# Expert rows turned by VectorE instead of TensorE, loaded in blocks; the expert tables moved into the branch

## The reference, cut to what matters

```python
x = attn_out.transpose(0, 2, 1, 3).reshape(3072, 512)
logits = x @ w_gate                    # 8 experts
expert_idx = np.argmax(logits, axis=1)
for e in range(8):
    mask = expert_idx == e
    h = np.maximum(x[mask] @ w1[e], 0.0)      # 512 -> 1024
    out[mask] = gate_w[mask, None] * (h @ w2[e])   # 1024 -> 512
h = out @ w_in                         # 512 -> 2048
g = (a0 + a1 h + a2 h^2 + a3 h^3) / (1 + |b0| |h| + |b1| h^2 + 1e-6)
y = g @ w_out                          # 2048 -> 512
```

## Time and profile before

| what | value |
|---|---|
| median of three runs | 1128.35 us |
| the profiled execution's own time | 1129.99 us |
| its span, first to last instruction | 1128.4 us |
| TensorE busy | 1095.0 us (97%) |
| VectorE busy | 896.5 us (79%) |
| ScalarE busy | 594.8 us (53%) |
| GpSimd busy | 259.7 us (23%) |
| mean granted TensorE clock | 0.995 of full speed |

### The profile page before, as it was taken

One profiled execution on the slowest core, in us unless ns is written; L12 is line 12 of the kernel. 1 busy time (PEld: TensorE's weight loads), 2 busy tenths in 40 slices (PEclk: granted clock), 3 DMA queues, 4 the chain that ended last, 5 costly groups with the idle time before them and its releaser, 6 DMA issues.

```text
span 1128.4 us, 19524 instructions
## 1 busy us (share of the span) xinstructions
PE 1095.0 (97%) x6023; PEld 890.5 (79%) x6024; DVE 896.5 (79%) x1810; ACT 594.8 (53%) x1063; POOL 259.7 (23%) x191
## 2 busy tenths in 40 slices
PE   6999999989999999999999999999999999999997
PEld 4677777678888888888887888888888888888885
DVE  5688788658878787878769987986986986996975
ACT  5788888422322222232338656655665655655663
POOL 1112111255646656563500001001001001000101
PEclk9999999899999999999999999999999999999999
DMA  8998861287757877975721010010002001000000
GB/s 196 310 240 215 225 169 59 71 280 262 269 193 274 278 249 240 305 233 201 258 94 49 1 39 38 1 38 37 0 0 76 0 0 64 12 0 10 28 1 38
DMA packets 142363, 142.54 MB, mean 126 GB/s; under 512 B 104672, under 2 KB 104672, under 8 KB 141280
## 3 DMA queue, kind: packets, MB, share of 16 engines
q0 software_dynamic: 27584, 92.48, 23.5%
q1 hardware_dynamic: 114720, 49.31, 16.3%
HBM read 118.70 MB, written 23.32 MB: 126 GB/s over the span
## 4 chain that ended last, share of the span: by engine, by line
PE 84%; DVE 8%; SPq 3%; DMA 2%; issue 2%; ACT 1%; POOL 0%; POOLq 0%; ACTq 0%; DVEq 0%
PE bank L1122 23%; PE bank L1124 23%; PE bank L1123 23%; PE bank L969 4%; PE bank L945 3%; PE bank L932 3%; DMA qraw<-in_q_dram 2%; PE bank L910 1%; PE bank L1117 1%; PE bank L985 1%; DVE poly L1726 1%; DVE poly L1724 1%; PE bank L1192 1%; DVE poly L1739 1%; SPq L316 1%
## 5 line engine op out<-in xcount | busy, mean ns | idle before, releaser
L1612 DVE STREAM_TRANSPOSE bank<-hbuf 32x256 f32<-32x256 f32 x464 | 211.6, 456 | 61.9 <-ACT hbuf L745 55.5
L469 POOL TENSOR_TENSOR w_lo<-stage,w_hi 128x2048 fp32r<-128x2048 f32 x32 | 147.6, 4614 | 64.9 <-DMA w_hi<-in_moe_w_dram 32.1
L1122 PE MATMUL bank<-w_hi,gh 128*128 128x512 f32 x384 | 150.5, 392 | 0.3 <-DVE gl L1748 0.3
L1122 PE MATMUL bank<-x2Th,w_hi 128*128 128x512 f32 x384 | 149.5, 389 | 0.5 <-DVE poly L1726 0.5
L1124 PE MATMUL bank<-w_hi,gl 128*128 128x512 f32 x384 | 149.5, 389 | 0.0
L1123 PE MATMUL bank<-w_lo,gh 128*128 128x512 f32 x384 | 149.4, 389 | 0.0
L1124 PE MATMUL bank<-x2Th,w_lo 128*128 128x512 f32 x384 | 149.4, 389 | 0.0
L1123 PE MATMUL bank<-x2Tl,w_hi 128*128 128x512 f32 x384 | 149.4, 389 | 0.0
L604 POOL DMA_INDIRECT out_dram<-stage,ids x24 | 29.6, 1235 | 510.1 <-ACT stage L854 494.3
L1122 PE MATMUL bank<-w_hi,xTh 128*128 (+1 forms) x248 | 96.7, 390 | 2.2 <-DVE xTl L1600 1.5
L756 ACT ACTIVATE ybuf<-bank 128x512 f32<-128x512 f32 x31 | 18.5, 598 | 149.8 <-PE bank L1124 141.8
(11 more groups left out here) (220 smaller groups left out, 2222.6 us busy)
## 6 DMA issues: line engine op xcount, KB each, us to landing
w_hi<-in_moe_w_dram POOLq DMA_DIRECT2D x32, 1024.0 KB, 7.8
stage<-in_moe_w_dram POOLq DMA_DIRECT2D x32, 1024.0 KB, 7.8
xg<-routed_x SPq DMA_DIRECT2D x31, 256.0 KB, 5.1
routed_y<-ybuf SPq DMA_DIRECT2D x31, 256.0 KB, 2.8
x<-routed_y SPq DMA_DIRECT2D x6, 1056.0 KB, 5.2
kraw<-in_k_dram SPq DMA_DIRECT2D x24, 256.0 KB, 5.1
qraw<-in_q_dram SPq DMA_DIRECT2D x24, 256.0 KB, 4.1
vraw<-in_v_dram SPq DMA_DIRECT2D x24, 256.0 KB, 4.1
```

Source lines behind the costliest of these rows:

```text
L469: pool.tensor_tensor(w_lo[:, at:at + CH], stage[:, c % 2, :], w_hi[:, at:at + CH].bitcast(F32), ALU.subtract).then_inc(chunk_ready, 1)
L1122: pe.matmul(dst, lhs_hi, rhs_hi, start=first, stop=False)
L1612: ins = dve.transpose(HB_ps[k][r * QD:(r + 1) * QD, :, q % 2 * QD:(q % 2 + 1) * QD], rows)
```

## The change

1. TensorE no longer turns x. VectorE does it with one `transpose` over 128x512, which turns each block of 32x32 within its 32 partitions. For this to be the whole turn, the loads place the blocks: each tile is loaded by four DMAs (`load_rows`), one for each group of 32 partitions, with four pieces of 128 columns per partition, and the columns of a row in `xs` stand in another order. `turn_x` writes them in that order (`quarters`), and the reciprocals of the sums are laid out to match it (`rcp` with 16 entries a tile, a `den` for the sums).
2. The turn of x of tile t+1 stands first in VectorE's `dve_tile(t)`. Tile 1 has places of its own (`XS_ps`, `xSh`, `xSl`).
3. The expert tables are a function, called at the end of each branch, and hold the turns of x0 and x1 and both low parts of x behind `tab_ready`. TensorE waits for `tab_ready` ahead of the up products of tile 0, and makes half of the up products of tile 1 before it turns h0. TensorE's loop has one tile per round, VectorE's two.
4. GpSimd waits for 64 instead of 16 at `xg_in[0]`.

```diff
+            def load_rows(r, row):
+                for a in range(4):
+                    sp.dma_start(xg[a * QD:(a + 1) * QD, r, :].rearrange("n (b c) -> n b c", b=4),
+                                 xs[ds(row, P), a * P:(a + 1) * P].rearrange("(b n) c -> n b c", b=4)).then_inc(xg_in[r], 16)
+
             def load_x(t, r, first=False):
...
-                sp.dma_start(xg[:, r, :], xs[ds(row, P), 0:DM]).then_inc(xg_in[r], 16)
+                load_rows(r, row)
...
-            moe_x(0)
-            moe_h(0); moe_x(1); end_ht(0, hTh)
+            moe_x(0); moe_x(1, XS_ps, xSh)
+            moe_h(0); end_ht(0, hTh)
...
+            def quarters(row, j):
+
+                return row.rearrange("p (a j n) -> p a j n", a=4, j=KB)[:, :, j, :]
...
-                    mm = pe.transpose(dst[:, j * P:(j + 1) * P], oT[:, i % 2, j, :], ident[:, :])
+                    mm = pe.transpose(quarters(dst[:, :], j), oT[:, i % 2, j, :], ident[:, :])
...
-            def moe_turn_x(r, n):
-
-                pe.wait_ge(xg_in[r], 16 * n)
-                for j in range(KB):
-                    mm = pe.transpose(X_ps[:, j * P:(j + 1) * P], xg[:, r, j * P:(j + 1) * P], ident[:, :])
-                mm.then_inc(xg_ps, 1)
...
-            def pe_tile(t, r, n):
+            def pe_tile(t):
...
-                moe_turn_x(r, n)
                 moe_down(t - 1, off_down, e_down)
                 moe_up(t + 1, off_up, e)
...
-            moe_turn_x(0, 1)
-            moe_up(0, 0, 0)
             pe.wait_ge(tab_ready, 1)
             off, e = weights_at(1), expert_of(1)
-            moe_turn_x(1, 1)
+            moe_up(0, 0, 0)
+            moe_up(1, off, e, xSh, xSl, (0,))
             turn_end_h(0)
-            moe_up(1, off, e)
-            pe_tile(1, 0, 2)
-            with pe.Fori(0, (MT - 3) // 2) as tp:
-                for r in range(2):
-                    pe_tile(2 * tp + r + 2, (r + 1) % 2, tp + r + 2)
+            moe_up(1, off, e, xSh, xSl, (1,))
+            pe_tile(1)
+            with pe.Fori(2, MT - 1) as t:
+                pe_tile(t)
...
-                dve.tensor_tensor(xt[:, i % QT, 0:DM].rearrange("p (h d) -> p h d", h=H),
-                                  src[:, :].rearrange("p (h d) -> p h d", h=H),
-                                  rcp[:, i % 2, 1, :].rearrange("p (h o) -> p h o", o=1).broadcast_to([P, H, D]),
+                dve.tensor_tensor(xt[:, i % QT, 0:DM].rearrange("p (s n) -> p s n", n=QD),
+                                  src[:, :].rearrange("p (s n) -> p s n", n=QD),
+                                  rcp[:, i % 2, :, :, :].rearrange("p u v (j o) -> p (u v j) o", o=1).broadcast_to([P, 16, QD]),
...
+            def turn_rows(t, r, n, dst=X_ps):
+
+                dve.wait_ge(xg_in[r], 64 * n)
+                if dst is X_ps and not (isinstance(t, int) and t == 0):
+                    dve.wait_ge(xg_lo, t)
+                dve.transpose(dst[:, :].rearrange("p (j b n) -> p j b n", j=KB, b=4),
+                              xg[:, r, :].rearrange("p (b j n) -> p j b n", j=KB, b=4)).then_inc(xg_ps, 1)
+
+            def expert_tables():
...
+                dve.tensor_copy(end_i[:, :, :], edge[:, 2:4, :]).then_inc(tab_ready, 1)
+                turn_rows(0, 0, 1); turn_rows(1, 1, 1, XS_ps)
+                moe_x(0); moe_x(1, XS_ps, xSh, xSl)
...
             with dve.If(banded(dve) > 0):
                 dve_steps()
+                expert_tables()
...
-            def dve_tile(t):
-                turn_h(t, 0); moe_x(t + 1); turn_h(t, 1); moe_ht(t)
-
-            moe_x(1); end_ht(0, hTh, hTl)
-            with dve.Fori(1, MT - 2) as t:
-                dve_tile(t)
+            def dve_tile(t, r, n):
+                turn_rows(t + 1, r, n); turn_h(t, 0); moe_x(t + 1); turn_h(t, 1); moe_ht(t)
+
+            end_ht(0, hTh, hTl)
+            with dve.Fori(0, (MT - 3) // 2) as tp:
+                for r in range(2):
+                    dve_tile(2 * tp + r + 1, r, tp + 2)
+            turn_rows(MT - 1, 0, MT // 2 + 1)
```

More of the change, by code:

```diff
@@ L139, in build_program @@
         sums = over("sums", [P, 2, H])
-        rcp = over("rcp", [P, 2, 2, H])
+        den = over("den", [P, 2, H])
+        rcp = over("rcp", [P, 2, 2, 2, KB])
         zeros = over("zeros", [P, RW])
@@ L163, in build_program @@
         early = free[1]
+        x2_at = free[1]
         x2 = over("x2", [P, G, RW])
+        xSh, x2_at = place("xSh", [P, KB, P], F32R, x2_at)
+        xSl, _ = place("xSl", [P, KB, P], F32R, x2_at)
         x2Th = over("x2Th", [P, KB, G * P], F32R)
@@ L194, in build_program @@
         HT_ps = bank[2:4]
+        XS_ps = bank[6]
         HB_ps = [bank[2 + k].rearrange("p (j n) -> p j n", j=FB) for k in range(2)]
@@ L675, in evac_logits, with head_cols @@
                 act.activation(lgT[:, :], X_ps[:, 0:P], ACT.Copy).then_inc(lt_sb, 1)
+            def head_cols(row, h):
+                return row.rearrange("p (u v j n) -> p u v j n", u=2, v=2, j=KB)[:, h % 2, :, h // 2, :]
             def normalise_last():
@@ L1124, in three, with moe_up @@
                 return pe.matmul(dst, lhs_lo, rhs_hi, start=False, stop=last)
-            def moe_up(t, off, e):
+            def moe_up(t, off, e, hi=xTh, lo=xTl, halves=(0, 1)):
                 pe.wait_ge(chunk_ready, e * 4 + 2)
                 pe.wait_ge(xg_lo, t + 1)
-                for n in range(2):
+                for n in halves:
                     if not isinstance(t, int) or t > 0:
@@ L1135, in moe_up @@
                         at = off + j * F + n * 512
-                        mm = three(H_ps[n][:, :], xTh[:, j, :], xTl[:, j, :], w_hi[:, ds(at, 512)], w_lo[:, ds(at, 512)],
+                        mm = three(H_ps[n][:, :], hi[:, j, :], lo[:, j, :], w_hi[:, ds(at, 512)], w_lo[:, ds(at, 512)],
                                    j == 0, j == KB - 1)
@@ L1563, in _ @@
                     low_part(n // 4, n % 4)
-            done[0] = 0
-            tl = lambda ins: link(ins, tab_step)
-            dve.wait_ge(count_ps, 1)
-            tl(dve.tensor_copy(expert_rows[:, :], X_ps[:, 0:E]))
-            per_tile = lambda x: x.rearrange("p (s o) -> p s o", o=1).broadcast_to([P, MT, E])
-            per_expert = lambda x: x.rearrange("p (o e) -> p o e", o=1).broadcast_to([P, MT, E])
-            tl(dve.tensor_tensor(more, expert_rows[:, :].rearrange("p (e o) -> p e o", o=1).broadcast_to([P, E, NT]),
-                                 steps[:, :].rearrange("p (o j) -> p o j", o=1).broadcast_to([P, E, NT]), ALU.is_gt))
@@ L1590, in _ @@
-            for k in range(2):
-                tl(dve.tensor_tensor(prod[:, k, :, :], past, per_expert(wide[:, 0, k, :]), ALU.mult))
-            tl(dve.tensor_reduce(ttab[:, 0:2, :], prod[:, 0:2, :, :], AX.X, ALU.add))
-            tl(dve.tensor_tensor(ttab[:, 0, :], ttab[:, 0, :], row_no[:, :], ALU.add))
-            tl(dve.scalar_tensor_tensor(out=ttab[:, 2, :], in0=ttab[:, 1, :], scalar=last_at[:, 0:1], in1=ttab[:, 0, :],
-                                        op0=ALU.add, op1=ALU.min))
```

100 lines of the change are left out of this document (57 added, 43 removed).

## The result

The changed kernel takes 1132.76 us (median of 17 runs, 1130.96 to 1136.04) where the kernel before takes 1129.2 us (17 runs on the same chip, 1126.42 to 1131.19). The ratio is 1.0035, 95% interval 1.0027 to 1.0042: slower by a third of a per cent. The prediction was 1119.2 us, faster by 0.8%. It is wrong, in size and in sign. The profiled execution took 1132.76 us, its span is 1130.8 us.

The account below looks back on a forecast made before the run. The prediction took TensorE, with no gap to fill, to bound the expert stage. Loop -13.0 us and start-up +3.8 us summed to -9.2 us, from a median of 1128.35 to 1119.2 us, range 1113.5 to 1125.5.

Parts of the forecast that it names:

- What bounds the kernel: Expert stage: TensorE is busy 342.5 of 343.0 us; time saved there counts only while no other engine ends later.
- The loop, TensorE: Expert loop: x's transposes leave TensorE, 27 at 0.48 us, -13.0 us; bounds -13.5 and -9.5.
- The loop, VectorE: Expert loop: one added 0.73 us transpose per tile fits VectorE's wait for relu, 10.37 of 10.87 us; costs nothing.
- the estimate of 1.24 us: VectorE's transpose of x: four times the skill's 311 ns per 128x128 bf16, which would leave VectorE no slack.
- The loads: Loop: four DMAs of 512 B pieces per x tile instead of one; x is read two periods later; costs nothing.
- Attention stage: Before the expert stage: another column order and 16 reciprocals for 8, at most 24 x 0.01 us on VectorE; nothing.
- The start-up: Routing to first down product: earlier tables, but x1's landing and half clock delay TensorE; +3.8 us, bounds -1.5 to +9.
- The end: Stage's end: removing the last transpose (x30) buys nothing, as TensorE already waits 0.43 us there for VectorE; 0 us.
- A: Start-up rival: the clock stays up or x1 comes early; -12 us, 1116 us; chance 0.17.
- B: Loop rival: VectorE sets the pace, by a 1.2 to 1.6 us transpose or thin 0.4 us slack; about 1124; chance 0.14.
- C: Start-up rival: VectorE's 4.25 us gap before the tables stays; total -4.5 us, 1124 us; chance 0.09.
- D: Loop rival: VectorE's transpose runs its four quadrants in turn, 3.74 us; +60 us, 1188 us; chance 0.07.

Follow-up runs that it names:

- e6: Changed kernel with TensorE's four value reads split around the down products and only 8 of 128 columns per block of x's low part computed in the loop; ratio 0.9931.
- e8: Changed kernel with split reads, x0's low part before x1's turn, weights behind x1, x's low part earlier among h's transposes, 20 fillers for 8; 1110.89 us, ratio 0.9865.
- e1: Changed kernel with the two values that only the up products need read behind the down products; ratio 0.9991 to the kernel before.
- e7: Changed kernel with one more, unused value read per tile on TensorE's sequencer, ahead of the down products; 1141.65 us, ratio 1.0129 to the kernel before.
- e12: Kernel before the change with one more, unused value read per tile on TensorE's sequencer, ahead of the transposes; 1137.18 us, ratio 1.0068.
- e10: Kernel before the change with TensorE's four value reads split over the two borders of a tile; ratio 0.9995.
- e2: Changed kernel with only 8 of 128 columns per block of x's low part computed in the loop, the rest left out; ratio 0.9984 to the kernel before.
- e11: Changed kernel with 56 instead of 8 filler products on TensorE in the last group, behind the branch; ratio 1.0033 to the kernel before.
- e5: The changed kernel itself, unaltered, run again on another call's chip; 1131.10 us, ratio 1.0043 to the kernel before.
- e3: Changed kernel in which VectorE, at the start of the expert stage, makes x0's low part before it turns x1; ratio 0.9991 to the kernel before.
- e9: Kernel before the change with only the expert tables, coef and x0's low part moved inside the branch, x still turned by TensorE; ratio 1.0018.
- e4: Changed kernel in which GpSimd starts the second expert's weight loads only when x1 has landed too; ratio 1.0007 to the kernel before.

## Why the prediction was wrong

*What bounds the kernel: right as far as it went.* TensorE had no gap to fill. But "only while no other engine ends later" was weighed with engines alone. The holder that turned up is a sequencer, whose work no busy share counts.

*The loop, TensorE: the step that failed.* "The transposes go", priced at 0.48 us each with 27 of them, -13.0 us, and at least -9.5. The transposes are worth 0.50 us a tile (e6, e8), so the price was right; the step from "they go" to "the period falls by their price" failed. 3.8 us came of 13.0. The sequencer's branch and four reads hold the down products (S: e1 gives back 0.17 us a tile; e7 and e12, against e10), and x's low part holds the up products (e2 gives back 0.12); both mended together give 0.38. The prediction asked what covers the work that is added, and never what the removed work had been covering. It also put at nothing, without a word, that TensorE's loop now branches in every tile instead of every second one, 0.4 us of the sequencer each time.

The Trainium skill ("Advanced Engine Details and Errata", Sequencer and Instruction Queues, Control Flow Timing) gives some 108 ns for a compare-and-branch; this trace has 213 ns. The Trainium skill ("DMA: Bandwidth & Descriptors", Latency and other measured facts) gives a floor of about 600 ns for a `tensor_load`; the trace has 0.30 us for the load, and about 0.7 us from one read to the next with the register operations around it. The measured numbers decide. Four reads by that figure would be an estimate of 2.4 us; by the trace, about 3. Either number, beside the 3.7 us which the trace of before shows between a branch and the last up product (341.6 to 345.24), would have been a reason to ask.

*The loop, VectorE: right, but for one operand.* 0.73 us predicted and measured, and the estimate of 1.24 us beside it was not borne out; the transpose stands in the wait for the relu, of which 0.7 to 1.0 us are left. The 0.4 us before the down products were more than enough (1.0 us in the tile shown). Only the up products' low part was not on the list.

*The loads: right in the loop.* No tile waits for an x there. *Attention stage: right*, nothing to see beyond its spread.

*The start-up: the steps right, one size off.* (Its sum is +3.6, not +3.8: 243.8 + 2.7 - 242.86. That changes nothing below.) Tables at once, row_i 5.5 us behind them (215.20 to 220.57 + 0.18), both low parts behind x1, the clock at its lower level, and 2.8 us lost by it (2.7 predicted; e11, though e5 lost 1.9). Missed: x1's landing. "I take 2.7 to 3" was 6.12 us. SP issued x1 8.6 to 10.5 us behind the last routing step (223.92 and 225.81, less 215.29), for 8.6 to 10.3 predicted. The weights were put at 10.2 us behind it and came at 9.6 (224.91 - 215.29), while x1 was still being issued, so the two collided as they do in the kernel before: the earlier trace rows showed 6.82 us for it, and I argued myself away from that row with a lead of a few tenths. x1's turn came 16.7 us after the last routing step (231.96 - 215.29) for 13.0 predicted, 3.7 us that cover the miss of 3.4 (+7.2 for +3.8).

*The end: 0.8 us where I had 0,* by the low part of the last x.

*The rivals.* A (clock up): no, 0.50. B (VectorE the pace): no; the loop's gain came a little below its lower end (-3.8 for -5 to -10), but neither of its two mechanisms is there: the transpose takes 0.73 us, and the low part of h is ready a microsecond early. VectorE did hold products, the up products, by the low part of x, which B doesn't name; that it was near in number is luck. C (the gap stays): no. D (3.74 us for the transpose): no. The result is slower than before, which I gave 0.08, and the mechanism that took the gain was in none of the rivals. Had x1 landed as predicted, the change would have been about even (+2.4 - 3.4 + 1.9 = +0.9 us in the profiled executions), not -9.2. Had the loop come as predicted and x1 late, it would still have been some 6 us faster (-9.2 + 3.4). So the error in the loop took the gain, and the one in the start-up made a loss of it.

## What to carry to other kernels

Before an operation is taken out of a saturated engine's stream, list what its duration may cover: the sequencer's branches, value reads and waits at that point, and every operand due right behind it; a profile without gaps says nothing of how near they are. Where two of them are near, neither mend alone shows its worth, so try them together. Put value reads behind the products that don't need them, and start bulk transfers behind the last small one that a critical step waits for.

## What the runs showed of the hardware

- One value read on TensorE's sequencer is a load of 0.30 us (least 0.296, most 1.1 over the loop), register operations of 0.05 and 0.15 and an assertion of 0.02, and about 0.7 us from one to the next. A branch is 0.21 us, and 0.4 us from its start to that of the next read.
- TensorE's sequencer ran only 3.4 to 3.7 us, 15 to 16 products with their weight loads, ahead of the products (branch at 446.9, last up product at 450.33; in e6 402.9 and 406.64; before the change 341.6 and 345.24). What sets this distance stays open.
- VectorE's transpose of 128x512 f32 takes 0.73 us with all partitions at once. One of 32x256 takes 0.47 (3.74 / 8), for an eighth of the elements.
- Behind the branch VectorE shows 4.25, 6.04 (e3) and 6.43 us (e9) of "issue", wherever the end of the branch falls in the program; the cause was not looked into.
- Four x loads of 64 KB landed within 1.80 us of the last issue without the weights beside them (e4), and within 6.12 us with them.
